# VectorE's sums of weights and blocks moved to the head of an item, and output copies moved behind an item's chain, in a one-core attention and two-layer kernel

## What is computed

```python
x = attention(q, k, v)                     # 2304 tokens x 512
h = x @ w_in                               # 512 -> 2048
x = np.where(h > 0, h, np.exp(np.minimum(h, 0)) - 1) @ w_out       # 2048 -> 512
g = x @ w_gate                             # 512 -> 1536
out = (g * (1 / (1 + np.exp(-g))) * (x @ w_val)) @ w_out2          # 1536 -> 512
```

## Time and profile before

| | |
|---|---|
| time, median of 3 executions | 981.39 us |
| the profiled execution's own time | 981.92 us |
| its span, first to last instruction | 980.0 us |
| TensorE matmul busy | 964.9 us |
| VectorE busy | 630.2 us |
| ScalarE busy | 386.1 us |
| GpSimd busy | 164.1 us |

### The profile page before, as it was taken

How to read it: one execution, slowest core, us unless ns; L and a number is a source line. 1 busy time by engine, 2 the same in 40 slices (tenths; PEclk the granted TensorE clock), 3 DMA queues, 4 the chain that set the end, 5 groups by cost and what they waited for, 6 DMA issues and landing times.

```text
span 980.0 us, 20203 instructions
## 1 busy us (share of the span) xinstructions
PE 964.9 (98%) x7903; PEld 912.7 (93%) x7904; DVE 630.2 (64%) x1424; ACT 386.1 (39%) x1026; POOL 164.1 (17%) x210
## 2 busy tenths in 40 slices
PE   8999999999999999999999999999999999999998
PEld 5989999999999999999999889999999899999998
DVE  7787656566555665655358586646768857768753
ACT  5677554344344444443335533232324421322211
POOL 7304420004000000000008720000009910000000
PEclk9799999999999999999999999999999999999999
DMA  9545431125111210210223201112023122120202
GB/s 246 181 122 112 96 63 47 27 74 103 29 37 32 72 51 26 63 34 6 77 86 108 76 11 56 43 46 65 1 87 129 60 93 87 43 86 22 87 1 86
DMA packets 55661, 67.88 MB, mean 69 GB/s; under 512 B 6760, under 2 KB 37832, under 8 KB 55568
## 3 DMA queue, kind: packets, MB, share of 16 engines
q1 hardware_dynamic: 48112, 62.67, 20.6%
q0 software_dynamic: 6816, 3.55, 2.7%
q10 hardware_dynamic: 640, 0.39, 0.2%
HBM read 52.42 MB, written 14.16 MB: 68 GB/s over the span
## 4 chain that ended last, share of the span: by engine, by line
PE 85%; DVE 6%; ACT 4%; issue 2%; DMA 2%; ACTq 0%; DVEq 0%; SPq 0%
PE bank L571 26%; PE bank L572 25%; PE bank L573 25%; PE bank L535 2%; PE bank L502 2%; PE bank L520 2%; PE bank L557 1%; ACT gv_hl L1114 1%; PE bank L511 1%; DMA w_raw<-w 1%; ACT u_sb L1155 1%; ACT weights L1108 1%; DMA q_sb<-qT 1%; DVE u_sb L922 0%; PE bank L545 0%
## 5 line engine op out<-in xcount | busy, mean ns | idle before, releaser
L571 PE MATMUL bank<-x_hl,gv_hl 128*128 128x256 f32 x768 | 218.7, 285 | 5.4 <-ACT p_sb L1137 3.3
L572 PE MATMUL bank<-x_hl,gv_hl 128*128 128x256 f32 x768 | 217.8, 284 | 0.0
L573 PE MATMUL bank<-x_hl,gv_hl 128*128 128x256 f32 x768 | 217.8, 284 | 0.0
L571 PEld LDWEIGHTS bank<-x_hl,gv_hl 128*128 128x128 f32 x768 | 147.8, 192 | 8.1 <-ACT p_sb L1137 4.4
L571 PE MATMUL bank<-x_hl,weights 128*128 128x384 f32 (+1 forms) x448 | 148.7, 332 | 2.4 <-DVE weights L790 1.7
L1309 POOL TENSOR_TENSOR gv_hl<-gv_raw,gv_hl 128x256 fp32r<-128x256 f32 x84 | 74.7, 924 | 455.8 <-ACT gv_hl L1114 455.8
L572 PEld LDWEIGHTS bank<-x_hl,gv_hl 128*128 128x128 f32 x768 | 147.8, 192 | 0.9
L573 PEld LDWEIGHTS bank<-x_hl,gv_hl 128*128 128x128 f32 x768 | 147.8, 192 | 0.0
L571 PE MATMUL bank<-g_hl,weights 128*128 128x384 f32 (+1 forms) x448 | 147.7, 330 | 0.0
L572 PE MATMUL bank<-x_hl,weights 128*128 128x384 f32 (+1 forms) x448 | 145.0, 324 | 0.0
L573 PE MATMUL bank<-x_hl,weights 128*128 128x384 f32 (+1 forms) x448 | 144.9, 323 | 0.0
(11 more groups left out here) (128 smaller groups left out, 1629.5 us busy)
## 6 DMA issues: line engine op xcount, KB each, us to landing
landing<-w SPq DMA_DIRECT2D x32, 256.0 KB, 4.1
x_raw<-yT_scratch SPq DMA_DIRECT2D x14, 512.0 KB, 4.3
v_win<-v_windows SPq DMA_DIRECT2D x46, 105.0 KB
q_sb<-qT SPq DMA_DIRECT2D x88, 48.0 KB, 2.2
partT_scratch<-out_sb SPq DMA_DIRECT2D x16, 256.0 KB, 2.0
out_sb<-partT_scratch SPq DMA_DIRECT2D x4, 1024.0 KB, 5.1
outT<-out_sb SPq DMA_DIRECT2D x16, 256.0 KB, 2.1
k_sb<-kT SPq DMA_DIRECT2D x14, 288.0 KB, 3.7
```

Of the source, the lines that this page charges most:

```text
L571: nc.tensor.matmul(out, w_hi, x_hi, start=first, stop=False)
L572: nc.tensor.matmul(out, w_hi, x_lo, start=False, stop=False)
L573: return nc.tensor.matmul(out, w_lo, x_hi, start=False, stop=last)
```

## The change

No instruction changes what it computes. In a wide item of the second layer:

- VectorE's weight sums (tensor j = 0 whole), block sums and the first two parts of the block lows come first in the item. The sums of tensor 1 are split around the sum u3, and the remaining block lows follow c11.
- `dve_out` comes behind the low parts of u. `act_out` comes behind the high parts of u and behind `act_p1` of the next item.

```diff
@@ VectorE's queue
                 if is_wide(v):
-                    dve_u2(dve, n)
-                    dve_u3(dve, n)
-                    dve_c22_u4(dve, n)
-                    dve_c11(dve, n)
                     for h, q in sums_of(v, p):
                         dve_sum_weights(dve, h, q, 0)
-                        dve_sum_weights(dve, h, q, 1)
                     if p == 1 and v + 1 in LOADED:
                         dve_sum_blocks(dve, v + 1)
                     if p == 2 and v + 1 in LOADED:
-                        dve_blocks_low(dve, v + 1, range(len(x_parts(v + 1))))
+                        dve_blocks_low(dve, v + 1, range(2))
+                    dve_u2(dve, n)
+                    for h, q in sums_of(v, p):
+                        dve_sum_weights(dve, h, q, 1, 0)
+                    dve_u3(dve, n)
+                    for h, q in sums_of(v, p):
+                        dve_sum_weights(dve, h, q, 1, 1)
+                    dve_c22_u4(dve, n)
+                    dve_c11(dve, n)
+                    if p == 2 and v + 1 in LOADED:
+                        dve_blocks_low(dve, v + 1, range(2, len(x_parts(v + 1))))
                     dve_c21(dve, n)
                     dve_gate(dve, n, 0)
                     dve_c12(dve, n)
                     dve_value(dve, n, 0)
                     dve_gate(dve, n, 1)
                     dve_value(dve, n, 1)
+                    dve_u_low(dve, n, 0)
+                    dve_u_low(dve, n, 1)
                     if p == 0 and v - 1 >= NT2:
                         dve_out(dve, v - 1)
-                    dve_u_low(dve, n, 0)
-                    dve_u_low(dve, n, 1)
@@ ScalarE's queue
                     act_sigmoid(act, n, 0)
                     act_sigmoid(act, n, 1)
-                    if p == 0 and 0 < v <= NT2:
-                        act_out(act, v - 1)
                     act_u_high(act, n, 0)
                     act_u_high(act, n, 1)
                     if n + 1 < len(ITEMS) and is_wide(ITEMS[n + 1][0]):
                         act_p1(act, n + 1)
+                    if p == 0 and 0 < v <= NT2:
+                        act_out(act, v - 1)
```

## The result

The changed kernel takes 986.85 us (median of 4 executions, 985.72 to 987.68) against 981.35 us before (4 executions): a ratio of 1.0056, 95% interval 1.0036 to 1.0077. It is 5.5 us slower; 988 was forecast.

A forecast was written before the change was run, and what follows sets the result against it. TensorE, 98% busy, was taken to bound the kernel, its standing worth 7 to 9 us. Items 13 to 16 (+6.3) and 0 to 2 (+0.2) gave 981.39 + 6.5 = 987.9, said as 988; range 986 to 990, 8-in-10 984 to 991.

The forecast's parts named there:

- the two places: Where TensorE stands in the second layer: items 0 to 2 (560 to 582 us) and items 14 to 16 (763 to 796).
- step 3: Recovery behind c21(13): VectorE is the bound, c12(15) starts 6.2 us later; lower end 4.3 if VectorE is not.
- items 0 to 2: Item 0's gain is spent ahead of u2(1), c21(1) starts unchanged, low clock adds 1.1: +0.2 us, -1.2 to +0.9.
- Step 1: Item 13: weight load (1,0) waits behind the output copies, is issued 3.4 us later and lands at 735.0.
- Step 2: Item 13: VectorE's sums need the load ahead of u2(13); TensorE stands 4.4 us at c21(13), then low clock, 1.2 us.
- Steps 4 and 5: Wait at c11(16) goes, -0.9 us; later w3(1,2) load lengthens the wait at c11(17), +1.0, or only +0.1.
- The rest: Other items of the second layer cost nothing: no TensorE waits between items 3 and 12 or behind 17.
- mild contention: Rival: VectorE not the bound behind c21(13), four sums nearer 1.6 us, item 1's block sums earlier: 984.4 us, chance 0.20.
- The heavier case: Rival: load (1,0) lands at 736.5 behind all four stores, or sums each wait out GpSimd: 990.5 us, chance 0.17.
- The other side: Rival: load (1,0) lands by 726, waits of items 14 to 16 go, -2.6 us, total about 979; chance 0.08.

The follow-up runs named there:

- Experiment 3: Changed kernel with SyncE's weight load (1,0) moved ahead of the four stores of visit 3: second layer 437.4 us.
- Experiment 4: Changed kernel with both loads, weights (1,0) and w3(1,2), moved ahead of the stores: second layer 436.3 us.
- experiment 7: Changed kernel with GpSimd filling the low parts of weights (0,2) and their w3 with zeros instead of subtracting: second layer 438.9 us.
- experiment 6: Changed kernel with the block sums back behind c11 and the first block lows still ahead of u2: second layer 439.2 us.
- experiments 2 and 9: Both on the kernel before. 2: only the output copies moved, second layer 442.5 us. 9: only both loads ahead of the stores, 436.4 us.

## Why the prediction was right

The direction, the size (5.5 us measured between medians, 6.5 forecast) and the two places were right. The bound that it assumed in step 3 was not, and its sum for items 0 to 2 lay outside its own range; the two errors have opposite signs. By its own steps, against the table of differences:

- **Step 1, the load.** Forecast 3.4 us later and 4.7 us to land; measured 3.4 us later relative to p1(13) (4.6 less 1.2), and 4.8 us:

```profile
gv_raw<-wg SPq DMA_DIRECT2D x1, 512.0 KB, 4.8
```

- **Step 2, the wait.** Forecast 4.4 us at c21(13), released by u2; measured a wait of 4.45 and a delay of 4.6, with 14 matmuls at the low clock behind it. Experiment 3 shows the cause by taking it away.
- **Step 3, the recovery.** Forecast +6.2 at c12(15), with VectorE as the bound from c21(13) on; measured +5.0. The assumed bound was wrong. The forecast has TensorE stand 1.9 us for u3 at c12(15) (772.85 against 771.0). It stood 0.06 us there and not at all in item 14, so VectorE came out level with TensorE and held nothing up. What makes the +5.0 is the 4.6 of step 2, and 0.4 since: c21(13) to c12(15) is 34.2 us, where experiment 3 without any wait or low clock takes 32.5 and the kernel before, with its 1.3 us of waits, took 33.8. That is the sum by which the prediction gave its lower end of 4.3. VectorE was faster than forecast because the four sums of item 14 took 2.5 us (750.11 to 752.65) instead of 3.0, and the pairs of sums behind u2 mostly 1.2 instead of 1.5 to 1.8; the four of item 15 took more, 3.5 (766.03 to 769.54) instead of 2.8:

```profile
750.11 0.95 DVE L832 TENSOR_TENSOR gv_raw<-gv_raw 128x256 f32<-128x256 f32 x1
751.09 0.84 DVE L834 TENSOR_TENSOR gv_raw<-gv_raw 128x256 f32<-128x256 f32 x1
751.86 0.41 DVE L838 TENSOR_TENSOR gv_raw<-gv_raw 128x256 f32<-128x256 f32 x1
752.31 0.42 DVE L840 TENSOR_TENSOR gv_raw<-gv_raw 128x256 f32<-128x256 f32 x1
752.65 0.68 DVE L881 TENSOR_TENSOR u_sb<-bank,p_sb 128x512 f32<-128x512 f32 x1
```

- **Steps 4 and 5.** Forecast -0.9 and +1.0; measured -0.7 and +1.0. Experiment 4 gave back 1.2 for the second load.
- **Items 0 to 2.** Forecast +0.2, at most +0.9; measured **+2.5**, outside its range. The mechanism held: the gain of item 0 was spent ahead of u2(1), and the wait at c11(2) went. (That wait was 0.84 us; the 1.1 us by which the prediction names it is the one at c11(1), which stayed, with 1.33.) Two terms were mis-sized. c21(1) came 1.3 us later than before rather than at the same time, since the chain of item 0 ended some 0.6 us later than I worked out (18.3 us behind p1(0) rather than 17.7) and the block sums took 4.5 us rather than at most 4.3. And the low clock cost 2.3 us instead of 1.1, because I gave it one product's length and it covered two.
- **The rest.** No wait of TensorE between items 3 and 12 or behind item 17, as forecast.

The two errors, -1.0 in items 13 to 17 and +2.3 in items 0 to 2, leave 1.3. Counted by the second layer the change cost 7.8 us, 1.3 more than the sum. The medians came out at 5.5, and their interval of 3.5 to 7.6 us holds the 6.5. That they lie nearer to the forecast than the second layer does is luck, as far as the profiled pair tells: there the start was 2.1 us earlier after the change, which the forecast knew nothing of. Whether it was earlier in the other executions too isn't known, since they have no trace.

Of the rivals, mild contention was right that VectorE is not the bound behind step 2, and wrong for item 1, whose block sums took 4.5 us. That contention sets the size there is shown by experiment 7. The heavier case didn't come: the load landed at 735.5, and four sums took 2.5 and 3.5 us rather than 3.8. The other side, a load that lands early enough, is what experiment 3 made: 6.8 us less than after. With it in place the kernel was at 437.4 us, so that even then it wasn't faster than before, because items 0 and 1 had lost what items 14 to 16 gained. The prediction had 2.6 us of gain in items 14 to 16 and a total of about 979. From p1(13) to the end experiment 3 gained 1.4, because c11(17) still waited 0.93 us for the second load; with that load early too (experiment 4) it gained 2.6. The rest of the miss is the error in items 0 to 2.

## What to carry to other kernels

Moving an instruction on one engine moves everything that waits for it in other queues, and there the next entry as well: four output copies on a mostly idle ScalarE held four stores, and the stores held a weight load of another stage behind them. Before preparation work is put at the head of a stage, ask when its data land and which short-term consumer stands behind it; here the right place for the block sums was right behind the sums that release TensorE's next banks, and for the loads ahead of the stores. The weight sums could stay at the head once their load was early. When two effects of one change have opposite signs, undo them separately: with the harmful parts corrected, the same idea made the kernel 0.7% faster than before.

## What the runs showed of the hardware that I had not expected

- After a wait of TensorE of about the same length the granted clock was low for 3.4 us or for 6.8 us: 3.4 behind 4.45 us at c21(13) in the changed kernel, 6.8 behind 4.40 us there in experiment 6, and 6.8 behind the 4.58 us at c21(1). So one wait of 4.5 us cost some 1.4 or 2.3 us on top, and which of them wasn't known beforehand. In the second layers of these twelve profiles every wait of 4.18 us or more had a low stretch behind it, and none of 1.64 us or less. Between them the same length went both ways: 1.99 us had one behind it in the kernel before and none in experiments 2 and 9, and of the waits of 2.2 to 2.3 us at c11(15) and c11(17) in experiment 2 only the second had one.
- A VectorE sum of 128x512 with both inputs in SBUF takes 0.69 us alone and 0.98 to 1.22 us beside GpSimd's subtractions, and again 0.69 beside GpSimd's fills.
- The first part of the kernel, the same in all, varies by 3.4 us between executions (p1(0) from 540.8 to 544.2), most of it in the first 40 us. For changes of under 1% a time counted from a fixed instruction inside one profile told more than the whole time.
